# First batch of a fused attention, MLP and gated-convolution kernel: value sums on GpSimd, and the splitting of the MLP weights moved

## What is computed

```python
# attention: a pooled part and a local part, added
q_d, k_d, v_d = (a.reshape(B, H, Sd, 4, D).mean(axis=3) for a in (q, k, v))   # 144 rows
out_up = np.repeat(softmax_attention(q_d, k_d, v_d), 4, axis=2)
mask = np.abs(pos[:, None] - pos[None, :]) < 4
out_local = softmax_attention(q, k, v, mask)
x = out_up + out_local                                     # -> [batch, 576, 512]
# mixing and MLP
u = x + real(fft(fft(x, axis=1), axis=2))
un = (u - mean(u)) / sqrt(var(u) + 1e-6)
x = u + maximum(un @ w_ch1, 0) @ w_ch2                     # 512 -> 2048 -> 512
# gated value
gate = sigmoid(causal_conv5(x, conv_w))
out = gate * (x @ w_val) @ w_out
```

## Time and profile before

| | |
|---|---|
| median of 3 runs | 819.88 us (819.36 to 827.78) |
| the profiled execution | 816.47 us |
| its span (first to last instruction) | 814.7 us |
| PE busy | 728.4 us, 89% |
| DVE, ACT, POOL busy | 436.8, 204.7, 65.3 us |
| HBM read and written | 43.38 MB, 4.72 MB |

### The profile page before, as it was taken

One profiled execution on the slowest core, in us unless ns is written; L12 is line 12 of the kernel. 1 busy time (PEld: TensorE's weight loads), 2 busy tenths in 40 slices (PEclk: granted clock), 3 DMA queues, 4 the chain that ended last, 5 costly groups with the idle time before them and its releaser, 6 DMA issues.

```text
span 814.7 us, 15570 instructions
## 1 busy us (share of the span) xinstructions
PE 728.4 (89%) x5956; PEld 542.8 (67%) x5956; DVE 436.8 (54%) x955; ACT 204.7 (25%) x409; POOL 65.3 (8%) x82
## 2 busy tenths in 40 slices
PE   1838546799999998999999998999999999999998
PEld 1624225577776776787776776777776777777776
DVE  6838769744453585644553584643643681113552
ACT  1206585222221122222221122222211122111101
POOL 3000213000110210000100210000100210000000
PEclk9999555999999999999999999999999999999999
DMA  9991031702200103602200204513100000000001
GB/s 285 285 254 46 2 130 54 170 9 71 62 1 1 59 30 105 127 12 75 48 1 1 59 30 131 104 29 79 26 2 1 0 30 30 2 1 1 1 15 45
DMA packets 42106, 49.15 MB, mean 60 GB/s; under 512 B 4784, under 2 KB 35568, under 8 KB 40944
## 3 DMA queue, kind: packets, MB, share of 16 engines
q1 hardware_dynamic: 33392, 31.69, 16.1%
q10 hardware_dynamic: 8640, 16.43, 6.2%
HBM read 43.38 MB, written 4.72 MB: 59 GB/s over the span
## 4 chain that ended last, share of the span: by engine, by line
PE 72%; DVE 11%; DMA 6%; issue 6%; ACT 3%; POOL 1%; SPq 1%; ACTq 0%; DVEq 0%; POOLq 0%
PE P L499 21%; PE Y L515 21%; PE P L622 4%; PE Y L611 4%; PE Y L622 3%; PE A L524 3%; DMA kl<-qk_win 2%; PE A L486 2%; DMA shared<-v_pool 2%; PE A L479 2%; PE A L469 2%; PE A L411 1%; PE A L572 1%; PE A L422 1%; PE A L566 1%
## 5 line engine op out<-in xcount | busy, mean ns | idle before, releaser
L499 PE MATMUL P<-unT,w 128*128 128x288 f16 x1536 | 210.0, 287 | 8.7 <-issue 4.8
L515 PE MATMUL Y<-hT,w 128*128 128x288 f16 x1536 | 214.9, 286 | 1.5 <-DVE xT L1068 1.5
L1047 DVE SCALAR_TENSOR_TENSOR hT<-P,hT 128x288 f16<-128x288 f32 x128 | 58.3, 456 | 259.1 <-ACT hT L728 259.1
L499 PEld LDWEIGHTS P<-unT,w 128*128 128x128 f16 x1536 | 148.4, 98 | 52.4 <-issue 12.2
L515 PEld LDWEIGHTS Y<-hT,w 128*128 128x128 f16 x1536 | 144.8, 98 | 45.6 <-issue 7.0
L728 ACT ACTIVATE hT<-P 128x288 f16<-128x288 f32 x128 | 52.5, 410 | 193.5 <-PE P L499 193.4
L1083 DVE SCALAR_TENSOR_TENSOR gate<-xT,cw,gate 128x288 f32<-128x288 f32 x128 | 66.4, 519 | 4.5
L699 ACT ACTIVATE prob_or_un<-prob_or_un 73x288 f32<-73x288 f32 (+1 forms) x52 | 23.3, 449 | 141.4 <-DVE prob_or_un L918 141.4
L524 PE MATMUL A<-sdft,pair_or_folded 128*128 128x289 f32 (+5 forms) x102 | 32.7, 443 | 8.7 <-DVE pair_or_folded L975 8.7
L622 PE MATMUL P<-shared,wo 128*128 128x288 f32 x128 | 32.1, 409 | 0.7 <-DVE shared L1095 0.5
L622 PE MATMUL Y<-shared,wo 128*128 128x288 f32 x128 | 32.1, 409 | 0.5 <-DVE shared L1095 0.5
(11 more groups left out here) (147 smaller groups left out, 831.4 us busy)
## 6 DMA issues: line engine op xcount, KB each, us to landing
w<-w_ch ACTq DMA_DIRECT2D x8, 1024.0 KB, 12.0
kl<-qk_win SPq DMA_DIRECT2D x40, 140.0 KB, 5.2
ql<-qk_win SPq DMA_DIRECT2D x20, 256.0 KB, 4.9
vl<-v_win SPq DMA_DIRECT2D x72, 65.0 KB
pair_or_folded<-qk_pool SPq DMA_DIRECT2D x8, 580.0 KB, 4.9
pair_or_spectrum<-qk_pool SPq DMA_DIRECT2D x8, 580.0 KB, 5.3
out<-ot ACTq DMA_DIRECT2D x32, 144.0 KB, 1.8
x<-v_pool SPq DMA_DIRECT2D x4, 576.0 KB
```

The lines of the kernel that those rows point to most:

```text
L499: last = mm(P[s % 2][:, 0:HN], w1s[:, k, f * 128:(f + 1) * 128, wt], unT[:, ut, k, ha * HN:(ha + 1) * HN], start=k == 0 and wt + ut == 0, ...
L515: last = mm(Y[d][:, 0:HN], w2s[:, f, d * 128:(d + 1) * 128, wt], hT[s % 3][:, ht, :], start=f == 0 and wt + ht == 0, stop=f == KF - 1 and ...
L1047: nc.vector.scalar_tensor_tensor(out=hT[s % 3][:, 1, :], in0=P[s % 2][:, 0:HN], scalar=0.0, in1=hT[s % 3][:, 0, :], op0=ALU.max, op1=ALU.s ...
```

## The change

Five things are done in the first batch, and nothing in the last two middle steps.

1. The two `pool_v` of the opening leave DVE. POOL does them as `first_values`: two additions for each half (1024 and then 512 elements for each partition), behind its fills with zeros. At the very start POOL also makes its constant -0.5 by adding -0.25 to itself.
2. The identity has a semaphore of its own (`ld_id`) and is loaded before the values; the other six constants are waited for only by the first local unit.
3. The loads of w_ch1 stand one ACT slot later, those of w_ch2 in slots 10 to 13 instead of 6, 7, 9 and 10, and the Fourier tables in slot 9.
4. `W1_AT` goes from 11 to 14: the maxima of w_ch1 stand in DVE's slots 8 to 11 instead of 5 to 8, and its splitting starts at ACT's slot 14. The maxima of w_ch2 come in one block behind the whole splitting of w_ch1.
5. Only the high and low parts of the first two chunks of w_ch2 are made at the end of the opening. The other six are split in slots 0 to 17 of the first middle step, which is now written out (`step(1, 0)`), and the loop does two steps instead of three.

```diff
-        POOLING_FIRST = {1: [("qk", 1)], 2: [("v", 0)], 3: [("v", 1), ("qk", 2)], 5: [("qk", 3)]}
-        WEIGHT_LOADS = [2, 3, 4, 5, 6, 7, 9, 10, 8]
+        POOLING_FIRST = {1: [("qk", 1)], 3: [("qk", 2)], 5: [("qk", 3)]}
+        WEIGHT_LOADS = [3, 4, 5, 6, 10, 11, 12, 13, 9]
-        W1_AT = 11
+        W1_AT = 14
-        CONSTS = 7 * 16
+        CONSTS = 6 * 16
...
                 if part == 0:
                     pe.wait_ge(hid_sb, n + 1)
                     if s == 0:
-                        pe.wait_ge(w_split, 2 * WCH)
                         pe.wait_ge(step_over, b + 1)
+                    if opening(b) and s < KF and s % 2 == 0:
+                        pe.wait_ge(w_split, WCH + s // 2 + 1)
...
                     if m is not None:
                         relu(m, s)
+                        if opening(m) and s % 2 == 0 and s < 2 * WCH:
+                            weights(WCH + 2 + s // 2)
...
                         hidden_low(m, s)
+                        if opening(m) and s % 2 == 1 and s < 2 * WCH - 4:
+                            weight_low(WCH + 2 + s // 2)
...
                 if m is None:
                     nc.vector.memset(xT[:, :, 0:TAPS - 1], 0.0)
-                    for c in range(WCH, WCH + 5):
+                    for c in range(S0 + NU + LAG_AV + 3 - W1_AT, WCH):
                         weight_low(c)
+                    for c in range(WCH, 2 * WCH):
+                        weight_max(c)
+                    weight_top(1)
+                    weight_scale(1)
                     combine(b, 0)
-                    weight_low(WCH + 5)
                     statistics(b, 0)
...
-                    weight_low(WCH + 7)
+                    weight_low(WCH)
+                    weight_low(WCH + 1)
...
+            def first_values(k):
+
+                half = vraw[k].rearrange("p (h r) c -> p h r c", h=2)
+                pool.wait_ge(ld_vraw[k], 16)
+                pt(half[:, 0], half[:, 0], half[:, 1], ALU.add).then_inc(v_half, 1)
+                pool.wait_ge(v_half, k + 1)
+                pt(vd[:, k, :, 0:D], half[:, 0, 0].rearrange("p (h c) -> p h c", h=H), half[:, 0, 1].rearrange("p (h c) -> p h c", h=H),
+                   ALU.add).then_inc(v_pooled, 1)
...
-            nc.gpsimd.memset(mv[:], 1.0)
-            nc.gpsimd.memset(mhalf[:], -0.5).then_inc(init, 1)
+            nc.gpsimd.memset(mhalf[:], -0.25).then_inc(quartered, 1)
+            pool.wait_ge(quartered, 1)
+            pt(mhalf[:], mhalf[:], mhalf[:], ALU.add).then_inc(quartered, 1)
+            nc.gpsimd.memset(mv[:], 1.0).then_inc(init, 1)
...
-            pool.wait_ge(ld_const, CONSTS)
+            first_values(0)
+            first_values(1)
+            pool.wait_ge(ld_id, 16)
...
-            with pe.Fori(0, B - 1) as it:
+            step(1, 0)
+            with pe.Fori(1, B - 1) as it:
                 step(it + 1, it)
```

45 lines of the change are left out of this document (23 added, 22 removed).

## The result

The changed kernel takes 823.75 us (median of 20 runs, 820.29 to 831.93) against 820.53 for the kernel before beside it. The ratio is 1.0051 with a 95% interval of 1.0032 to 1.0071, so it is 2.6 to 5.8 us slower. A second measurement of the same kernel, later in the study, gave 1.0074 [1.0045, 1.0103]. The forecast was 0.9 us faster. The time lies inside the range, the sign does not. The profiled execution took 825.24 us (span 823.0), 8.3 us of span above the one of before.

What follows compares the result with a forecast made beforehand. PE was taken to bound the kernel, with winnable time only in the opening's some 140 us. Terms -6.5 + 6.2 - 2.3 + 4.0 - 2.3 = -0.9 us gave 819.0 us against a median of 819.88, range 811 to 827.

Steps and rivals of the forecast that it cites:

- The start: Kernel's opening: POOL's first ISA row costs 7.3 us, first unit with values at 23.5 us, third keys still issued at 40.8.
- the ISA rows are cheap: Rival, chance 0.18: POOL's pause is paid once or its code is already there; `mix_rev` 5.4 us sooner, 810 us in all.
- The third keys: Keys of the third local unit, in the opening: land 12.6 us after issue, at 53.4 instead of 59.1, 5.7 us won.
- The other local units: Opening's later local units: 2.0 us won from ACT's copies, 1.2 lost on the fifth unit's keys.
- T: End of the third local unit's copy, from which the mixing starts: 70.6 us forecast, 6.5 earlier than 77.06.
- From T to `mix_rev`: End of the opening: 49.0 us instead of 42.8, 6.2 lost to eight late maxima and POOL's uncovered ISA row.
- Up to the MLP: From `mix_rev` to the MLP's start: `weight_low` no longer holds the statistics and last normalising, 2.3 us won.
- The first middle step: Splitting beside the MLP: +1.8 us before `hidden_low`, +2.2 from slots 1 and 3, nothing from slot 5 on; 4.0 lost.
- The listed sign: Forecast fails if PE waits on ACT or DVE in later slots of the first middle step.
- The loop: Middle steps' loop: PE idles 4.8 us at two turns back; one turn less wins 2.3 us (0 to 2.5).
- the four rivals: Cheap ISA rows 810 us (0.18), early keys 812 (0.12), lasting DMA contention 826 (0.16), late value sums 825 (0.08).

Runs made afterwards that it cites:

- the maxima earlier: Changed kernel with each maximum of w_ch2 behind a weight_low of w_ch1 instead of all eight in one block: 815.59 us, 0.995 of the kernel before.
- The small addition: Kernel before with a 128x2 GpSimd addition into a spare place right behind the first all-reduce: 814.46 us, ratio 0.9926.
- The load in the slots alone: Kernel before with step(1, 0) written out and the changed kernel's splitting instructions there on other data, results thrown away: 821.86 us, 1.004 (its base 0.9986).
- the best version of the whole change: Changed kernel with maxima behind each weight_low and a small addition behind the first all-reduce: 813.34 us, 0.9925; with splits also at their slots' ends 813.18 us, 0.9924.

## Why the prediction missed

Step by step, in the order of its own sum.

**The start.** The price of 7.3 us for GpSimd's first library row was wrong; it cost 0.30 (1.13 us). The prediction took one pause, seen behind an all-reduce, for a price of the first call. The runs show a pause where GpSimd goes from an all-reduce to an addition, and one ahead of an all-reduce at the program's start, but none ahead of an addition there. It moved little: the values were 6.3 us sooner than forecast (17.23 against 23.5), and with the sums back on VectorE the time is the same. The third keys were issued at 38.49 instead of 40.8, although PE had been ready for them at 34.51. The prediction had PE's scores alone as what they wait for; SyncE's own issuing of the values ended last, at 38.37. The rival that this belonged to ("the ISA rows are cheap") was half right and came to nothing: its keys were to be issued near 34, and the second pause stayed at 6.87.

**The third keys.** Forecast 53.4, used at 51.96, 52.34 in the second execution. The size was right, partly by luck. The forecast had the same issue and a landing in 12.6 us; the issue came 2.3 us sooner and the landing took 13.5. And the profile before was a late one: against the four executions with that opening (58.0 at the mean) the gain is 5.8 us. That the order of loads is the cause is shown by the run with the old order, which brings 57.41 and costs 4 to 7 us.

**The other local units, T.** Forecast 70.6, measured 72.12 and 70.57. That the second figure fits is luck: the keys came 1.1 us sooner than forecast there, and the term behind them was 1.0 too small. From the third keys to T it took 20.2 and 18.2 us, where the profile before had 18.0 and the forecast 17.2. ACT's copies gave the 2.0 us back as forecast (the copy now stands 1.5 us behind its matmuls, before 3.4). The fifth unit's keys cost nothing; no wait stands before their use at 64.51. What was left out is PE's pace: in the profile before it rose some 8 us behind the first use of the third keys, in the second profile of the changed kernel 13 us behind it, and in the first not before T (32 matmuls at 77.43 still took 1.94 us). The kernel before shows 18.0, 18.0, 18.0 and 20.2 us for the stretch, so this is scatter between executions as well.

**From T to `mix_rev`.** Forecast 49.0, measured 49.8 and 50.1 with pauses of 6.87 and 7.00. The loss of 6.2 us was right in kind and 1 us too small (42.8 before): eight maxima in a row, and the pause without cover. It is the largest term that was forecast as a loss, and the edit that undoes it, the maxima earlier, is worth 8 to 10 us, more than everything the change had won. The small addition undoes something else, the pause ahead of the first addition of x, which the kernel before has as well.

**Up to the MLP.** 2.3 us forecast; from `mix_rev` to the MLP it took 17.89 us against 20.31, 2.4 won. So the opening as a whole ended at 139.81 and 138.50, against 140.17 before (138.61 to 140.46 in the four profiles with that opening, 139.6 at the mean): some 0.5 us won by the change, where 2.6 were forecast.

**The first middle step.** This is the step that failed. 4.0 us were forecast; the profiles show 83.7 and 81.9 us from the MLP's start to the fills of x, against 75.9, 76.2 and 77.4 in the three of the kernel before and its version with one turn less: 4.5 to 7.8 lost, 6.3 by the means. In three parts:

- Up to slot 4 some 2.2 us (19.46 and 18.94 from the MLP's start, against 16.05, 17.38 and 17.55), where 1.8 were forecast. The run with the six chunks left out has it too (19.85), so it comes from the two `weight_low` at the opening's end: `hidden_low` came 9.25 us behind the MLP's start instead of 7.6 to 7.9. The slow twelve matmuls behind it (3.06) are no mark of the change; a version of the kernel before has them too.
- In slot 4 another 2.2 us (7.84 and 7.99 us, against 5.12, 6.08 and 6.08). This is the chain that the prediction had at 2.2: `weight_low` in slots 1 and 3, the shift, the exponential, `unit_av`. It gave only part of it as waiting, 1.74 us instead of 0.43 to 1.40; the rest is slower matmuls behind the wait, which the sum didn't have.
- From slot 5 on 1.2 and 2.7 us (54.95 and 56.40, against 53.7 in all three). The prediction put this at nothing: DVE's and ACT's work "stays under" PE's slot, "so no more is lost". But the four slots with a `weight_low` are 0.2 to 0.4 us longer each, 1.2 in all, since `weight_low` delays `xd` on DVE, for which PE waits. In the first profile the twelve matmuls of slot 5 took 3.09 us on top of that.

So the term that was put at nothing measured 1.2 to 2.7 us, and that is most of the 2.3 by which this step missed. Both later parts go when the splits leave the slots. The granted clock agrees: in 160 to 180 us it was 0.83 and 0.91 in the changed kernel and 1.00 in the three others. The load in the slots alone costs 2.8 to 4.0 us of distance, where the prediction had 2.2. The listed sign, PE waiting on ACT in later slots, is no clear mark of this: a wait for probT of 1.40 us was there before.

**The loop.** Forecast 2.3 won, measured 1.0 [-0.6, 2.5] and 1.2 [-1.1, 3.4], and with the splits in the opening 0 to 1. The row of PE's wait was right, but the pause was counted in full, and nothing asked who used it: in the timeline it is spent within five slots. The intervals don't exclude 2.3; the stretch behind the fills shows no gain.

Together, with the means of the profiles (four with the opening of before, three for the middle step, two of the changed kernel):

| | forecast | before | changed | difference |
|---|---|---|---|---|
| T | -6.5 | 76.5 | 71.3 | -5.1 |
| T to `mix_rev` | +6.2 | 42.8 | 49.9 | +7.2 |
| `mix_rev` to MLP | -2.3 | 20.4 | 17.9 | -2.5 |
| MLP to fills of x | +4.0 | 76.5 | 82.8 | +6.3 |
| the turn | -2.3 | | | 0 to -1.2 |

That gives 4.7 to 5.9 us, and the two measurements of the changed kernel gave 4.2 and 6.1. The sum of the forecast was a small difference of large terms of both signs, so misses of 1 to 2 us in each decided the sign, with the middle step's 2.3 the largest. None of the four rivals came about.

The edits add up only roughly. In the frame of the changed kernel the later loads give 4 to 7 us, the splits in the middle step 5 to 7, the sums on GpSimd 0; the maxima put behind all of this cost 8 to 10.

## What to carry to other kernels

Where GpSimd goes from an all-reduce to additions, look for some 7 us without a releaser, and put a tiny addition at a moment when the engine is idle; here that one edit of the kernel before is worth as much as the best version of the whole change. A pause of the bounding engine is not a gain to be had in full: ask which engine caught up in it. Work that is taken off one stage and laid beside a stage "with room" must be judged by the order on each engine's queue, by what it stands ahead of and the bounding engine waits for next (here the shift and `xd`, behind 1.4 us of VectorE's splitting), not by the engine's busy share. And where a transfer is to be asked for sooner, look at what its queue has to issue ahead of it (here loads of values until 38.37 us).

## What the hardware showed

- GpSimd's pause is tied to the change of function and not to the first call: from all-reduce to addition 7.32, 7.04, 6.87, 7.12, 7.00, 7.63 and 7.81 us in the runs above, from the program's start to an all-reduce 9.62, from the start to an addition 0.30. From an addition to a later all-reduce GpSimd waits for VectorE anyway (23.61 us in the changed kernel), and no pause can be seen. The Trainium skill, "GPSIMD Engine Reference", section "Instruction dispatch", gives about 6 us (5.95) for the first call to freshly loaded code; the rows from all-reduce to addition are 0.9 to 1.9 us longer, and the pause comes again ahead of additions that had run before. That it is a loading of code is the page's reading; the rows show only the pause.
- A fill of 128x6144 on GpSimd (5.21 us) stretched two instructions of VectorE from 0.99 to 5.86 us.
- The same 32 matmuls, those of the fourth local unit, took 1.94 us in the changed kernel's first profile (at 72.65) and 1.10 in the second (at 70.26), with a granted clock of 1.00 in the stretch of both; the granted clock alone doesn't show the slower pace. The two stretches:

```profile
72.00:76.00 4.00, 4.00 (x39) 2.26 (x40) 0.69 (x1) 1.54 (x3) 1.03 (x2) 1.00 0.01 2
```
```profile
68.00:72.00 4.00, 3.63 (x64) 2.21 (x54) 2.59 (x12) 2.58 (x5) 1.03 (x2) 1.00 0.01 2
```
